# RWKV outputs in strips of 32 columns written straight into the dense layer's input, two units moved into the dense stage

## What is computed

```python
for t in range(S):
    kt, vt, rt = (k[:, :, t], v[:, :, t], r[:, :, t])
    cur = np.einsum('bhd,bhe->bhde', u[None] * kt, vt)
    y[:, :, t] = np.einsum('bhd,bhde->bhe', rt, state + cur)
    state = w[None, :, :, None] * state + np.einsum('bhd,bhe->bhde', kt, vt)
```

## Time and profile before

| what | value |
|---|---|
| runs | 882.27, 878.20, 877.39 us; median 878.2 |
| profiled execution | 878.01 us; span of its instructions 876.1 us, so 1.9 us lie around the span |
| mean granted TensorE clock | 0.987 |
| TensorE busy | 845.8 us, 97% of the span |
| VectorE, ScalarE, GpSimd busy | 543.1, 314.5, 175.5 us (62%, 36%, 20%) |
| chain that ended last | TensorE 90%, DMA 3%, VectorE 3% |

### The profile page before, as it was taken

How to read it: one execution, slowest core, us unless ns; L and a number is a source line. 1 busy time by engine, 2 the same in 40 slices (tenths; PEclk the granted TensorE clock), 3 DMA queues, 4 the chain that set the end, 5 groups by cost and what they waited for, 6 DMA issues and landing times.

```text
span 876.1 us, 16448 instructions
## 1 busy us (share of the span) xinstructions
PE 845.8 (97%) x6107; PEld 740.7 (85%) x6107; DVE 543.1 (62%) x1063; ACT 314.5 (36%) x500; POOL 175.5 (20%) x141
## 2 busy tenths in 40 slices
PE   7699999999999999999999999999799999999995
PEld 6578888888888888878788878899799999999995
DVE  8677746564566445644443445566878777887770
ACT  1233223111311131112211221456267766677651
POOL 3533302242133303230101001003121101111010
PEclk9799999999999999999999999999899999999998
DMA  9763420342024302330011003457497678766700
GB/s 363 256 215 134 144 96 16 87 167 65 0 74 146 110 1 65 117 117 1 10 46 38 1 1 120 170 207 231 183 410 275 235 259 320 251 252 247 277 17 19
DMA packets 37282, 125.78 MB, mean 144 GB/s; under 512 B 4236, under 2 KB 21056, under 8 KB 31600
## 3 DMA queue, kind: packets, MB, share of 16 engines
q1 hardware_dynamic: 32848, 108.14, 35.0%
q0 software_dynamic: 3520, 9.87, 2.9%
q10 hardware_dynamic: 864, 7.08, 2.3%
HBM read 107.26 MB, written 18.88 MB: 144 GB/s over the span
## 4 chain that ended last, share of the span: by engine, by line
PE 90%; DMA 3%; DVE 3%; issue 1%; POOL 1%; ACT 1%; SPq 0%; ACTq 0%; POOLq 0%; DVEq 0%
PE bank L1599 33%; PE bank L1645 6%; PE bank L1647 6%; PE bank L1646 6%; PE bank L1698 4%; PE bank L1696 4%; PE bank L1697 4%; PE bank L1677 4%; PE bank L1678 4%; PE bank L1679 4%; PE bank L1674 3%; PE bank L1540 2%; PE bank L1522 2%; PE bank L1535 1%; PE bank L1500 1%
## 5 line engine op out<-in xcount | busy, mean ns | idle before, releaser
L1599 PE MATMUL bank<-X1H,WH 128*128 128x512 f32 x432 | 169.1, 391 | 1.4 <-DVE YS L1003 1.1
L1599 PE MATMUL bank<-X1L,WH 128*128 128x512 f32 x432 | 168.2, 389 | 0.0
L1599 PE MATMUL bank<-X1H,WL 128*128 128x512 f32 x432 | 168.2, 389 | 0.0
L1238 DVE TENSOR_TENSOR TT<-bank,SG 128x512 f32<-128x512 f32 x72 | 49.7, 691 | 132.3 <-ACT SG L802 132.2
L802 ACT ACTIVATE SG<-bank 128x512 f32<-128x512 f32 x72 | 43.0, 597 | 237.6 <-PE bank L1599 237.6
L732 ACT ACTIVATE AH<-PP 128x512 fp32r<-128x512 f32 (+1 forms) x78 | 46.1, 598 | 157.8 <-DVE PP L1243 155.6
L1599 PEld LDWEIGHTS bank<-X1H,WH 128*128 128x128 f32 x432 | 81.1, 188 | 19.8 <-issue 2.8
L1599 PEld LDWEIGHTS bank<-X1H,WL 128*128 128x128 f32 x432 | 81.1, 188 | 17.1
L1599 PEld LDWEIGHTS bank<-X1L,WH 128*128 128x128 f32 x432 | 81.1, 188 | 16.5
L1645 PE MATMUL bank<-AH,WH 128*128 128x512 f32 (+1 forms) x234 | 91.5, 391 | 0.0
L1647 PE MATMUL bank<-AH,WL 128*128 128x512 f32 (+1 forms) x234 | 87.8, 375 | 0.0
(11 more groups left out here) (229 smaller groups left out, 1805.7 us busy)
## 6 DMA issues: line engine op xcount, KB each, us to landing
W_EVEN<-w SPq DMA_DIRECT2D x20, 1536.0 KB
W_ODD<-w SPq DMA_DIRECT2D x18, 1536.0 KB, 7.7
RK_IN<-unit_rk SPq DMA_DIRECT2D x18, 736.0 KB, 5.5
V_IN<-unit_v SPq DMA_DIRECT2D x18, 448.0 KB, 3.5
STG<-w_dense ACTq DMA_DIRECT2D x6, 1152.0 KB, 6.3
mixed<-YS SPq DMA_DIRECT2D x40, 96.0 KB, 2.1
X<-mixed SPq DMA_DIRECT2D x5, 768.0 KB, 4.4
XG_ODD<-store SPq DMA_DIRECT2D x9, 394.0 KB, 8.3
```

What stands on the lines that cost most here:

```text
L1238: tt(TT[:, :], GATE_PS[:, :], SG[:, :], ALU.mult).then_inc(gate_free, 1)
L1599: last = mm(bank_[:, :], lhs[:, f, m, k * P:k * P + P], rhs[:, k, :], start=(x == 0), stop=(x == len(terms) - 1))
```

## The change

- The weights' columns and the output partitions of the RWKV matmuls are cut into strips of 32. An even head's 48 columns are padded to 64 behind, an odd head's in front, so that a pair of heads fills three strips, the middle one with the end of one head and the beginning of the other added up. `key_sums` and both halves of `outputs` so have 16 matmuls of at most 32 weight columns instead of 8 of 48 or 64. The 12 strips are the 3 tiles of X1, in an order (STRIPS) by which the rows of `w_gate` and `w_val` are permuted on the host.
- VectorE's `own_key` and `add_output` write X1 itself. `mixed`, YS, `store_output`, `load_x1` and the waits on them are gone. For units 0 to 3 each is one instruction of 128x384, for the others four of 128 or 64 partitions by 128 columns instead of two of 112x256.
- Only units 0 to 3 stand before the dense stage; 4 and 5 go into block 0 with 6 and 7, and every block up to 4 has four units. Their first loads are issued by ScalarE's queue beside SP's.
- For units 0 to 3 the keys by token are neither loaded nor scaled on GpSimd: TensorE transposes the scaled keys KW (`turn_keys`, 4 transposes), ScalarE copies them (`turned_keys`), and the missing factor is put on the first state (`first_state`, 4 small ScalarE instructions instead of 1). Unit 3's keys and receptances are scaled by GpSimd, those of units 0 to 2 by VectorE. A sigmoid of 8 columns loads ScalarE's table early.
- The first `up` of block 0 takes all high products first, then low inputs, then low weights, and waits for each kind by itself.
- YO and IDX have a copy per buffer, `out_written` is one semaphore per buffer. The experts of the late tiles are worked out before their rows (`plan_experts`), and SP loads late tile 0's weights then, before its rows.

```diff
-HEAD_AT = ((0, 1, 2, 3), (5, 4, 7, 6))
+STRIP = 32
+STRIPS = (((0, 0), (0, 2), (0, 1)), ((1, 0), (0, 3), (1, 1)), ((1, 2), (2, 0), (1, 3)), ((2, 2), (2, 1), (2, 3)))
...
+LOWER = [Piece(h, i) for h, i in ((0, 0), (1, 1), (0, 1), (2, 1), (2, 0), (3, 1), (1, 0), (3, 0))]
+UPPER = [Piece(h, i) for h, i in ((4, 0), (5, 1), (4, 1), (6, 1), (6, 0), (7, 1), (5, 0), (7, 0))]
+BOTH = [p for four in ((LOWER, 0), (UPPER, 0), (LOWER, 4), (UPPER, 4)) for p in four[0][four[1]:four[1] + 4]]
...
     def units_of_block(n):
-        late = isinstance(n, int) and n == CH - 2
-        return [Unit(n + 1, 2), Unit(n + 1, 3)] + ([] if late else [Unit(n + 2, 0), Unit(n + 2, 1)])
+        return [Unit(n + 1, b) for b in range(BATCH)]
...
             def own_key(u):
...
-                for x in range(2):
-                    cols = slice(HALF_COLS * x, HALF_COLS * (x + 1))
-                    last = tt(u.ys[:, cols], u.v[0:PR, I_VT:I_VV][:, cols], u.c_banks[x][0:PR, cols], ALU.mult)
+                if u.first:
+                    last = tt(X1[:, :, u.out], u.v[:, I_VT:I_VV].rearrange("p (k t) -> p k t", k=KT),
+                              u.c[:, 0:DM].rearrange("p (k t) -> p k t", k=KT), ALU.mult)
+                else:
+                    low, high = u.c_banks
+                    tt(X1[:, 0, u.out], u.own(0), low[:, 0:P], ALU.mult)
+                    tt(X1[LEFT, 1, u.out], u.own(1, LEFT), low[LEFT, P:2 * P], ALU.mult)
+                    tt(X1[RIGHT_, 1, u.out], u.own(1, RIGHT_), high[RIGHT_, P:2 * P], ALU.mult)
+                    last = tt(X1[:, 2, u.out], u.own(2), high[:, 2 * P:3 * P], ALU.mult)
...
             def set_index(tile):
-                need(dve, out_written, 16 * tile.before)
+                need(dve, out_written[tile.buffer], 16 * tile.of_buffer)
...
+            def plan_experts(q):
+                q.step(tt(TA[:, :, :], TB[:, :, :], by_entry(CST[:, C_EXP:C_EXP + 2 * NE], both), ALU.mult))
+                q.step(nc.vector.tensor_reduce(ETF[:, :], TA[:, :, :], AX.X, ALU.add))
+                nc.vector.tensor_copy(ETI[:, :], ETF[:, :]).then_inc(experts_ready, 1)
...
             set_index(tile)
             plan_entries(plan)
+            plan_experts(plan)
...
+                opened = set()
+                for p in pieces:
+                    a, at = p.head, (p.head.x, p.out.start)
+                    last = mm((u.c if u.first else u.c_banks[a.x])[p.out, p.cols], SELU[a.rows, a.s, p.cut], u.rxk[a.rows, a.keys],
+                              start=(pieces is not UPPER and at not in opened), stop=True, skip_group_check=True)
+                    opened.add(at)
...
+            turn_keys(u0)
             scores(u0)
+            turn_keys(u1)
             scores(u1)
...
-            key_sums(u0, STRAIGHT)
+            key_sums(u0, LOWER)
             outputs(u0)
-            key_sums(u0, CROSSED)
-            key_sums(u1, STRAIGHT)
+            key_sums(u0, UPPER)
+            scores(u2)
+            key_sums(u1, LOWER)
             outputs(u1)
-            key_sums(u1, CROSSED)
-            scores(u2)
+            key_sums(u1, UPPER)
+            scores(u3)
+            key_sums(u2, LOWER)
+            outputs(u2)
+            key_sums(u2, UPPER)
+            turn_keys(u2)
             state_terms(u0)
-            key_sums(u2, STRAIGHT)
+            key_sums(u3, LOWER)
+            outputs(u3)
+            key_sums(u3, UPPER)
+            turn_keys(u3)
             state_terms(u1)
-            key_sums(u2, CROSSED)
-            scores(u3)
-            outputs(u2)
...
```

More of the change, by code:

```diff
@@ L639, in scale_r @@
             def scale_r(u):
-                if u.start:
+                if u.first:
                     pool.wait_ge(scores_ready, 2 * u.i - 2)
@@ new lines, in x1_high_part @@
+            def x1_high_part(b):
+                act.wait_ge(y_added, b + 1)
+                part = Unit(0, b).out
+                copy(X1H[:, :, part], X1[:, :, part]).then_inc(*((x1_part_high, 1) if b < BATCH - 1 else (x1_high, KT)))
+            act.wait_ge(decays_loaded, 16)
+            act.wait_ge(select_zeroed, 1)
+            for odd in range(2):
+                last = copy(SELU[:, odd:PAIRS:2, (VW - HD) * odd:(VW - HD) * odd + HD],
+                            ucol[:, odd:PAIRS:2].unsqueeze(2).broadcast_to([PR, PAIRS // 2, HD]))
@@ L1024, in add_output @@
                 dve.wait_ge(c_used, u.i + 1)
-                for x in range(2):
-                    cols = slice(HALF_COLS * x, HALF_COLS * (x + 1))
-                    last = tt(u.ys[:, cols], u.y[x][0:PR, cols], u.ys[:, cols], ALU.add)
+                if u.first:
+                    last = tt(X1[:, :, u.out], u.y[:, 0:DM].rearrange("p (k t) -> p k t", k=KT), X1[:, :, u.out], ALU.add)
+                else:
+                    low, high = u.y
+                    tt(X1[:, 0, u.out], low[:, 0:P], X1[:, 0, u.out], ALU.add)
+                    tt(X1[LEFT, 1, u.out], low[LEFT, P:2 * P], X1[LEFT, 1, u.out], ALU.add)
+                    tt(X1[RIGHT_, 1, u.out], high[RIGHT_, P:2 * P], X1[RIGHT_, 1, u.out], ALU.add)
+                    last = tt(X1[:, 2, u.out], high[:, 2 * P:3 * P], X1[:, 2, u.out], ALU.add)
                 last.then_inc(y_added, 1)
@@ L1524, in scores, with turn_keys @@
                             last.then_inc(scores_ready, 1)
+            def turn_keys(u):
+                if u.b < 2:
+                    pe.wait_ge(k_start_scaled, u.i + 1)
+                else:
+                    pe.wait_ge(masked, 2 * u.i + 2)
+                for s in range(PAIRS):
+                    last = nc.tensor.transpose(u.keys_turned[:, s * PR:s * PR + PR], u.kw[:, s * P:s * P + P], ident[0:PR, 0:PR])
+                last.then_inc(keys_turned, 1)
             def outputs(u):
@@ L1527, in outputs @@
                 pe.wait_ge(masked, 2 * u.i + 2)
-                if u.start:
+                opened = set()
+                if u.first:
                     need(pe, tables_ready, u.i if u.i == 1 else 0)
                     need(pe, y_added, u.i - 1 if u.i in (2, 3) else 0)
-                if not u.first:
+                else:
                     pe.wait_ge(state_ready, u.i - BATCH + 1)
                     pe.nop(nofuse=True)
-                    for a in BY_QUARTER:
-                        mm(u.y[a.x][a.out:a.out + HD, a.cols], ST[a.rows, u.b, a.s, :], u.rw[a.rows, a.keys],
-                           start=(a.j % 2 == 0), stop=False, skip_group_check=True)
@@ L1537, in outputs @@
-                u.wait_v(pe)
-                for a in IN_ORDER:
-                    width = 64 if u.first and a.g == 0 else HD
-                    last = mm(u.y[a.x][a.out:a.out + width, a.cols], u.v[:, I_V + a.h * HD:I_V + a.h * HD + width],
-                              u.am[:, a.x, a.s, :], start=u.first, stop=(u.first or a.j % 2 == 1), skip_group_check=True)
+                    for p in BOTH:
+                        a, at = p.head, (p.head.x, p.out.start)
+                        mm(u.y[a.x][p.out, p.cols], ST[a.rows, u.b, a.s, p.cut], u.rw[a.rows, a.keys],
+                           start=at not in opened, stop=False, skip_group_check=True)
+                        opened.add(at)
@@ L1542, in outputs @@
+                u.wait_v(pe)
+                for p in LOWER + UPPER:
+                    a = p.head
+                    last = mm((u.y if u.first else u.y[a.x])[p.out, p.cols], u.v[:, a.v:a.v + VW][:, p.cut],
+                              u.am[:, a.x, a.s, :], start=u.first and p.out.start not in opened, stop=True, skip_group_check=True)
+                    opened.add(p.out.start)
                 last.then_inc(y_ready, 1)
             def state_terms(u):
-                pe.wait_ge(kt_scaled, u.i + 1)
+                if u.first:
+                    pe.wait_ge(kh_copied, u.i + 1)
+                    pe.wait_ge(masked, 2 * BATCH if u.odd else 2 * BATCH - 2)
+                else:
+                    pe.wait_ge(kt_scaled, u.i + 1)
@@ L1736, in dense_block @@
                             ranks(n)
-                    if first and f == 0:
-                        outputs(u5)
-                        state_terms(u5)
                     if f // 2 < len(units):
```

515 lines of the change are left out of this document (223 added, 292 removed).

## The result

The changed kernel takes 887.6 us (median of 4 runs, 885.52 to 887.7), the kernel before 878.1 in the same comparison: ratio 1.0096, 95% interval 1.0069 to 1.0123. It is slower, where I forecast 865. The profiled execution has a span of 885.7 us, 9.6 more than before.

The account below looks back on a forecast made before the run. TensorE, 97% busy, was taken as the bound through its idle time, clock and work. 878.0 - 16.0 (start) + 8.4 (units 4 and 5) + 1.6 (strips) - 7.4 (expert stage) = 864.6, forecast 865 us, range 858 to 873.

Parts of the forecast that it names:

- The strips: RWKV matmul groups: eight tiles run together, only group heads grow, some 0.08 us a unit, plus 1.6 us.
- The rival of 889 us: RWKV matmul groups: strips don't run eight at a time, L1500 and L1535 take twice as long, plus 24 us; chance 0.04.
- Units 4 and 5: Dense stage: block 4 gets four units instead of two, 4.2 us each, nothing covers it, plus 8.4 us.
- The first dense matmul at 28.0: Start: 14.6 us of TensorE work after GpSimd's first product gives 27.6, with short waits 28.0 us, instead of 42.80.
- so 11.7 us: Start: VectorE has scaled units 1 and 2 by then, four more products of 0.65 us after 9.09.
- 13.0 us: Start: GpSimd's first product, 1.27 us long, ends then, 0.6 us worse than before.
- I take 8.0 us: Block 0: from first dense matmul to second slice, instead of 9.24 us; bounds 6.5 and 9.5.
- granted clock 1.00 up to 60 us: Start and first dense slices: expected sign in the changed profile, where the clock was 0.61 from 30 to 43 us.
- a rival for the lower clock in the start: Start: waits between small groups lower the clock, the last 8 us of small work take 16, total 873 us; chance 0.08.
- From the second slice on, everything is TensorE's work: Dense stage: TensorE alone sets slice times; VectorE, 62% busy over the span, has room in every slice.
- Minus 7.4 in the expert stage: Expert stage: an index buffer per parity removes 5.1 us of wait, and lower-clock time falls from 4.7 to 2.4 us.
- My third rival: Expert stage: late rows land late or scatters hold VectorE, so the 6 us wait returns, total 871 us; chance 0.06.

Follow-up runs that it names:

- best1: The changed kernel with late rows loaded before late weights, TensorE's dense-block loop written out, and outputs added before the state's decay: 877.3 us, ratio 0.9981.
- quiet: best1 with the work of block 0's first slice reordered on GpSimd, ScalarE and VectorE, none left out: 883.2 us, ratio 1.0028.
- opening: quiet_warm with block 0's second slice reordered like the first, and GpSimd's scatters sent only after own_key of a block's fourth unit: 871.6 us, ratio 0.9912.
- filler: best1 with twelve matmuls nobody reads put into TensorE's gap in block 0's first slice: 883.0 us, ratio 1.0022.
- best1_again: best1 unchanged, run again as control in another group: 879.9 us, ratio 0.9985 to the kernel before.
- add_first: The changed kernel with outputs added into X1 ahead of the state's decay instead of behind it: 884.2 us, ratio 1.0044.
- drop_middle: The changed kernel without the four half-tile instructions per unit for X1's middle tile from unit 4 on (output not the reference's): 880.3 us, ratio 1.000.
- pe_unrolled: The changed kernel with TensorE's loop over dense blocks 1 to 3 written out: 885.5 us, ratio 1.0056.
- two_copies: The kernel before with only the index and output buffers in two copies: 872.3 us, ratio 0.9924.
- rows_first: The changed kernel with late tile 0's rows loaded ahead of its weights: 889.1 us, ratio 1.0103.
- two_again: two_copies unchanged, run again beside opening: 872.6 us, ratio 0.9912 to the kernel before.
- first_slice: The changed kernel with two of block 0's first three weight low parts behind the first product, and ScalarE's next load later: 893.7 us, ratio 1.0141.
- quiet_warm: quiet with 18 transposes of the identity at the start instead of 30: 879.2 us, ratio 0.999.

## Why the prediction was wrong

- **What bounds it: right.** TensorE was the bound, and what was lost is idle time, lower clock or more work on TensorE (busy 854.3 us instead of 845.8). Two of the three signs of being wrong came: a first dense matmul after 31 us, and new waits in the list.
- **The strips: right, sized a little low.** Eight tiles run at once. Of the 0.16 to 0.26 us by which a slice with outputs and state terms grew, the groups' heads are one part (32 records instead of 16 in L1519: 1.01 us to the next group, 0.91 before) and the state terms another (L1535 has 64 columns where 48 were: 0.68 us instead of 0.61). I had 0.08 a unit; it is about 0.2, some 4 us over 20 units instead of 1.6. By my estimate from TensorEngine Tiling (Array Packing) of the Trainium skill, section Performance Considerations (Instruction Overhead), each unit would have become 1.2 us longer; the 0.67 us for 32 records disagree. The rival of 889 us had nearly the right number for a reason that didn't occur.
- **Units 4 and 5: right.** Block 4 is 7.8 us longer (forecast 8.4).
- **The first dense matmul at 28.0: it failed at "so 11.7 us" and "13.0 us".** I counted VectorE's six products as a chain of their own and took the shared queues at 0 us. In the trace they wait for unit 1's load (0.94 us) and for unit 0's scores (1.47), which the 30 transposes hold back. GpSimd's first product so ended at 16.6, 3.6 us late, and the first dense matmul came at 32.3. With 18 transposes it came at 30.1, 1.3 us ahead of best1's.
- **"I take 8.0 us" for the first slice: it failed as an order, not as an amount of work.** It was 11.5. The 8.0 are there (quiet, opening: 8.01), but only if ScalarE's sigmoid doesn't stand behind a wait for VectorE's low parts and GpSimd doesn't work beside them. The first needs a wait of 2.8 us that my 8.0 did not hold, the second makes a low part 2.04 us instead of 0.95. I named both ("ScalarE comes to the first sigmoid later", "GpSimd scales unit 4 only once the low parts are there"; it was X1's low parts and not the weights') and priced neither.
- **"granted clock 1.00 up to 60 us": it failed.** I had a rival for the lower clock in the start, with 0.08 and 8 us; it came from the two gaps of the first slice and took 2.7 us in the next (filler and opening show that TensorE's gaps there are the cause). In the start itself it fell in some executions only: best1_again's profile has 0.50 from 25 to 30 us and its first dense matmul at 34.9, where best1's has 31.4.
- **"From the second slice on, everything is TensorE's work": it failed in blocks 1 to 4.** I wrote that VectorE has room in every slice. It has, by its sum. But the decay, on 256 columns instead of 192, takes 2.6 us in the median (1.4 before) and stood ahead of the four adds (1.9 us, add_first), and the half-tile instructions stand on the path from one block to the next (1.6 us, drop_middle).
- **Not seen at all:** the loop's end. Three of the five small groups in TensorE's body have 32 matmul records where they had 16, and its branch takes 3.3 us instead of 0.2. The two ends cost 3.3 us together (pe_unrolled).
- **Minus 7.4 in the expert stage: right as a mechanism.** Alone it gives 7 to 8 us (two_copies). The part that failed is "about 6 us earlier than today's 625.19": the rows were asked for at 631.17, behind a plan that the change cuts in two, and behind the weights, where they took 7.88 us to land. With the lower clock behind the wait this stage fell 4.4 us short, of which rows_first's trace gives 4.0 back. My third rival, "late tile 0's rows land late behind the weights", had a chance of 0.06 and the whole 6 us; it came in part.

Put together, the changed kernel in a better order (opening) has minus 13.3 us up to the third slice, plus 12.6 in the blocks and minus 6.4 behind them: 869.0 us of span. Against the forecast's minus 16.0, plus 10.0 and minus 7.4 that lacks 2.7, 2.6 and 1.0 us. The span is 16.7 us less than the changed kernel's 885.7, out of the 22.6 that separate the median from the forecast: most of the miss was order, with a loop and 12 transposes. Yet two_again, the smallest part of the change on the kernel before, is as fast (872.6 us, and 871.6 for opening, in one group): the rest is worth nothing measurable even in that order, since the blocks, with units 4 and 5 in the dense stage, pay back what the start gains.

**Left open:** what the pause of VectorE ahead of `own_key` is. It was there in the first and the third group and not in the second and fourth, and the first and fourth ran on the same chip; so it is neither the chip nor the kernel alone. It costs 3 to 4 us a kernel in the first group and 5 to 6 in the third. Why the clock falls in the start in some executions (first_slice and best1_again, whose code up to there is that of others without it) wasn't tried by itself. It is a good part of the scatter: of best1_again's ten runs the five with a mean clock of 0.985 to 0.988 took 880.8 to 882.6 us, the five with 0.991 to 0.993 took 877.6 to 879.0.

## What to carry to other kernels

When a long wait goes, price what was done in its shadow: before, while X1 went through memory, GpSimd's products and the splitting of the dense weights cost TensorE little; with X1 there earlier they stood ahead of the first sigmoid, or slowed what did, and became TensorE's wait, and the clock fell with it. Lay out every engine's queue in order, with the durations that its neighbours give it, and not its sum of busy time. And time the parts of a change one by one: the smallest one held all of the gain. Where one execution differs from the next by 3 us or more, compare several traces before a part is priced.

## What the runs showed of the hardware

- VectorE's instructions whose operands are both in SBUF slow down beside GpSimd's: 128x768 in 0.95 us alone and 2.04 beside it, the decay of 112x256 in 0.42 (once in quiet_warm, three times in opening), in 1.5 to 1.7 (add_first) and in 2.5 to 2.6 (the changed kernel), and GpSimd's product in 1.27 and 2.0. Those that read a bank (TT, PP, the adds) keep their times: TT takes 0.68 to 0.69 us all 72 times.
- Eight tiles of 48x32 run side by side: 32 matmul records in 0.67 us, 7 ns from start to start within a round of eight.
- With the longer body, the end of TensorE's loop has two packets of the instruction queue (none before) and a branch of 3.3 to 3.5 us (0.24 at most before), of which 1.5 us stay as TensorE's idle time.
- Rows of 394 KB that wait in a queue behind 3 MB of weights land 7.9 us after they are asked for, and 2.95 us ahead of them (the changed kernel, rows_first).
- The clock fell to 0.50 and 0.58 with idle gaps of 2.7 and 1.2 us that had small matmuls between them, and was low for some 10 us. A single gap of 1.8 us (opening) left it at 1.00.
